# Attention and feed-forward kernel: transposes one step late, ninth blocks of two tiles together, inverse sums turned by VectorE and spread by DMA

## The reference

```python
q_pool = q.reshape(B, H, S // 2, 2, D).mean(axis=3)
scores = scale * np.matmul(q_pool, k.transpose(0, 1, 3, 2))
attn = np.exp(scores - np.max(scores, axis=-1, keepdims=True))
attn = attn / (np.sum(attn, axis=-1, keepdims=True) + 1e-09)
x = np.matmul(attn, v)                      # then (B*S/2, H*D)
h = x @ w_in
out = (np.maximum(h, 0.0) + alpha * np.minimum(h, 0.0)) @ w_out
```

## Time and profile before

| | us |
|---|---|
| median of 3 runs | 931.72 |
| the profiled execution | 932.26 |
| its span, first to last instruction | 929.7 |
| TensorE busy | 887.3 |
| VectorE busy | 516.9 |
| ScalarE busy | 423.4 |
| GpSimd busy | 213.3 |

### The profile page before, as it was taken

One profiled execution on the slowest core, in us unless ns is written; L12 is line 12 of the kernel. 1 busy time (PEld: TensorE's weight loads), 2 busy tenths in 40 slices (PEclk: granted clock), 3 DMA queues, 4 the chain that ended last, 5 costly groups with the idle time before them and its releaser, 6 DMA issues. The chain is left out here.

```text
span 929.7 us, 20770 instructions
## 1 busy us (share of the span) xinstructions
PE 887.3 (95%) x6896; PEld 623.2 (67%) x6896; DVE 516.9 (56%) x836; ACT 423.4 (46%) x963; POOL 213.3 (23%) x182
## 2 busy tenths in 40 slices
PE   3799999999999999999999999999999999999997
PEld 1455555555555555555545799989999999989995
DVE  2676767677767776767676344344444444343442
ACT  2566666666666666666666222222322222322222
POOL 2112111211121112111200323323232323323230
PEclk9999999999999999999999999999999999999999
DMA  7435423542354235523520122212422222322211
GB/s 186 106 83 135 119 65 82 133 121 63 82 133 123 60 82 133 127 57 82 133 71 1 59 68 58 67 62 63 136 57 68 57 68 61 132 59 66 65 36 68
DMA packets 36366, 79.57 MB, mean 86 GB/s; under 512 B 5360, under 2 KB 9456, under 8 KB 36336
## 3 DMA queue, kind: packets, MB, share of 16 engines
q1 hardware_dynamic: 33936, 74.48, 31.0%
q10 hardware_dynamic: 2400, 4.72, 1.5%
HBM read 74.46 MB, written 4.72 MB: 85 GB/s over the span
## 5 line engine op out<-in xcount | busy, mean ns | idle before, releaser
L432 DVE TENSOR_REDUCE neg_max<-s_ps 128x1 f32<-128x1152 f32 x144 | 194.1, 1348 | 16.6 <-DVEq L431 16.6
L573 PE MATMUL pv_ps<-pt,v_f 128*64 128x256 f32 (+1 forms) x1152 | 169.0, 414 | 0.0
L532 PE MATMUL s_ps<-k_f,q_f 64*128 64x512 f32 (+1 forms) x640 | 160.2, 626 | 5.2 <-PEq L543 5.2
L348 ACT ACTIVATE e_sb<-s_ps,neg_max 128x1024 f32<-128x1024 f32 x144 | 160.1, 1112 | 0.0
L587 PEld LDWEIGHTS slot_ps<-ident,e_sb 64*128 64x128 f32 x2304 | 86.0, 139 | 82.4 <-issue 82.4
L465 DVE COPY pt<-slot_ps 128x512 f32<-128x512 f32 x144 | 99.6, 692 | 61.3 <-DVEq L464 59.4
L341 ACT ACTIVATE e_sb<-s_ps,neg_max 128x128 f32<-128x128 f32 x144 | 52.9, 367 | 171.5 <-ACTq L340 171.5
L617 PE MATMUL slot_ps<-x_hi,wi_hi 128*128 128x384 f32 x384 | 129.5, 337 | 1.1 <-PEq L613 1.1
L617 PE MATMUL slot_ps<-x_lo,wi_hi 128*128 128x384 f32 x384 | 129.5, 337 | 0.0
L617 PE MATMUL slot_ps<-x_hi,wi_lo 128*128 128x384 f32 x384 | 129.0, 336 | 0.0
L479 DVE TENSOR_SCALAR e_sb<-slot_ps,alpha_sb 128x384 f32<-128x384 f32 x96 | 59.3, 618 | 123.2 <-DVEq L477 123.2
(11 more groups left out here) (46 smaller groups left out, 1098.8 us busy)
## 6 DMA issues: line engine op xcount, KB each, us to landing
q_raw<-in_q SPq DMA_DIRECT2D x64, 288.0 KB, 4.5
k_f<-in_k SPq DMA_DIRECT2D x64, 288.0 KB, 4.2
wi_raw<-in_w_in SPq DMA_DIRECT2D x48, 256.0 KB, 2.6
wo_raw<-in_w_out SPq DMA_DIRECT2D x48, 256.0 KB, 2.6
v_f<-in_v SPq DMA_DIRECT2D x32, 288.0 KB, 3.0
out<-pt ACTq DMA_DIRECT2D x6, 768.0 KB, 4.4
k_end<-in_k SPq DMA_DIRECT2D x64, 32.0 KB, 4.0
alpha_sb<-in_alpha SPq DMA_DIRECT2D x1, 8.0 KB, 4.7
```

The costliest lines, as they stand in the source:

```text
L348: nc.scalar.activation(e_sb[:, b * NKEY + at:b * NKEY + at + n], s_ps[:, S_AT[b] + at:S_AT[b] + at + n], ACT.Exp, bias=neg_max[:, b:b + 1] ...
L432: nc.vector.tensor_reduce(out=neg_max[:, b:b + 1], in_=s_ps[:, S_AT[b]:S_AT[b] + NKEY], op=ALU.max, axis=AX_X, negate=True).then_inc(max_r ...
L532: ins = nc.tensor.matmul(s_ps[to:to + m, S_AT[b] + at:S_AT[b] + at + BANK], q_f[2 * g + h][rows, first:first + m], k_f[2 * g + h][rows, at ...
L573: ins = nc.tensor.matmul(pv_ps[h * D:(h + 1) * D, 0:n], v_f[2 * g + h][:, a, :], pt[:, a, at:at + n], start=(a == 0), stop=(a == KT - 1))
```

## The change

Each point is a part of the diff.

- TensorE transposes tile s-1 in step s, before it waits for the exponentials of tile s, so only the big scores stand behind that wait. `e_sb` holds three tiles. One more step (s = 144) transposes the last tile.
- The ninth blocks of tiles s-1 and s, and the small scores of tiles s+2 and s+3, are made in even steps, one after the other, and copied by one VectorE copy of 256 columns. In odd steps the product follows the big scores. The maximum of an odd step also waits for the first exponential of the tile before (`even_cut_done`). Block 8 has its own place (`pt_last`) and comes first in each product; the products begin a step later.
- `spread_inverse` and ScalarE's copy of its result are gone. VectorE turns the inverse sums in blocks of 32; SyncE stores them to a DRAM tensor `sums` in four pieces, waits for these, and loads them back to 64 partitions for each head, in two transfers per group. `scale` stands at t = 1 and 6.
- `scale` writes unsplit `x_f`. `x_hi` and `x_lo` hold the 768 tokens of a pass: made by GpSimd for pass 0 after 14 pairs, and by ScalarE (`x_high`) and VectorE (`x_low`) in the last block f of a pass for the next one. The first weights are rounded one step earlier.

The core of the diff; where old lines only go, or stand in the listing above, there is a line of dots.

```diff
-    SOURCE = [[(0, 0, P, 0)], [(1, 0, P, 0)], [(0, P, P, 0)], [(1, P, P, 0)],
-              [(0, 2 * P, HALF, 0), (1, 2 * P, HALF, HALF)],
+    SOURCE = [[(0, 0, P, 0)], [(1, HALF, P, 0)], [(0, P, P, 0)], [(1, HALF + P, P, 0)],
+              [(0, 2 * P, HALF, 0), (1, 0, HALF, HALF)],
...
-    PT_AT = [0, 320, 128, 448, 256, 640, 896, 768, 1024]
-    PT_MIX = 576
+    PT_AT = [0, 384, 128, 512, 256, 640, 896, 768, 1024]
+    SUM_AT = [0, 3, 1, 4, 2, 5, 7, 6, 8]
     GROUPS = [(0, 320, 320, 0), (640, 896, 256, 320)]
     GROUP_TILES = [(0, 5), (5, 9)]
-    PRODUCT = {5: (0, (0, 1)), 6: (0, (2, 3)), 7: (0, (4, 5)), 8: (0, (6, 7, 8)),
-               0: (1, (0, 1)), 1: (1, (2, 3)), 2: (1, (4, 5)), 3: (1, (6, 7)), 4: (1, (8,))}
-    SPREAD = {6: 0, 1: 1}
-    INVERT = {4: 0, 8: 1}
-    FIRST = 6
+    PRODUCT = {6: (0, (8, 0)), 7: (0, (1, 2)), 8: (0, (3, 4)), 0: (0, (5, 6, 7)),
+               1: (1, (8, 0)), 2: (1, (1, 2)), 3: (1, (3, 4)), 4: (1, (5, 6)), 5: (1, (7,))}
+    INVERT = {5: 0, 0: 1}
+    SCALE = {1: 0, 6: 1}
+    FIRST = 7
...
-        e_sb = sb("e_sb", [P, 2 * NKEY])
+        e_sb = sb("e_sb", [P, 3 * NKEY])
         pt_flat = sb("pt", [P, KT * 2 * NQ])
...
+        pt_last = pt_flat[:, 0:2 * NQ]
+        pt = pt_flat[:, 2 * NQ:].rearrange("p (a c) -> p a c", a=KT - 1)
         neg_max = sb("neg_max", [P, 2])
         row_sum = sb("row_sum", [P, 2, TILES])
         sum_eps = sb("sum_eps", [P, TILES])
...
+        inv_sum = sb("inv_sum", [P, 32])
+        inv_t = [sb(f"inv_t{i}", [P, 32]) for i in range(2)]
+        inv_bc = sb("inv_bc", [P, NQ])
...
+        x_f = sb("x_f", [P, DT * NTOK])
+        ff = sb("ff", [P, 11776], F32R)
...
+            for s in range(FIRST, REST + 1):
...
+            def store_sums(group):
+                a, b = GROUP_TILES[group]
+                sp.wait_ge(inv_turned, 1).then_inc(inv_turned, -1)
+                for i in range(0, P, 32):
+                    sp.dma_start(sums[a * P:b * P].rearrange("(t p) -> t p", p=P)[:, i:i + 32],
+                                 inv_t[group][i + a:i + b, :]).then_inc(inv_stored, 16)
+            def spread_sums(group):
+                _, _, n, first = GROUPS[group]
+                sp.wait_ge(inv_stored, 64).then_inc(inv_stored, -64)
+                for h in range(2):
+                    row = sums[GROUPS[group][h]:GROUPS[group][h] + n]
+                    sp.dma_start(inv_bc[h * D:(h + 1) * D, first:first + n],
+                                 row.rearrange("(o n) -> o n", o=1).to_broadcast([D, n])).then_inc(inv_bc_in[group], 16)
+            def sums_and_qk(pair, g):
+                store_sums(0)
                 load_q(pair * 2)
+                spread_sums(0)
                 sp.wait_ge(k_free[g], 1).then_inc(k_free[g], -1)
                 load_k(pair * 2, 2 * g), load_k(pair * 2 + 1, 2 * g + 1)
+                store_sums(1)
                 load_q(pair * 2 + 1)
...
+                spread_sums(1)
...
+            sums_and_qk(2, 0)
+            with sp.Fori(0, NPAIR // 2 - 2) as two:
                 for g in range(2):
...
+                    sums_and_qk(two * 2 + 3 + g, 1 - g)
+                    load_v_pair(two * 2 + 2 + g, g)
...
+            def x_split(h):
+                nc.gpsimd.tensor_copy(x_part(x_hi, h), x_chunk(0, h)).then_inc(pool_self, 1)
+                pool.wait_ge(pool_self, 1).then_inc(pool_self, -1)
...
+            pool.wait_ge(x_done, NPAIR - 2)
+            x_split(0), x_split(1)
...
+                    exponential_cut(s + 1, exp_cut_done if s % 2 == 0 else even_cut_done)
+                if s > 0:
+                    act.wait_ge(tr_ready[0], 1).then_inc(tr_ready[0], -1)
+                    nc.scalar.activation(pt_half((s - 1) % TILES, 0), half_columns(slot_ps[0][:, :]),
+                                         ACT.Copy).then_inc(slot_free[0], 1)
                 if left > 0:
                     exponential(s + 1)
...
+                elif left == 0:
+                    wi_high(0)
...
+            def x_high(n, h):
+                nc.scalar.activation(x_part(x_hi, h), x_chunk(n, h), ACT.Copy).then_inc(x_hi_done, 1)
...
+            def scale(group, pair):
                 _, _, n, first = GROUPS[group]
...
+                dve.wait_ge(inv_bc_in[group], 32).then_inc(inv_bc_in[group], -32)
                 dve.wait_ge(pv_done, 2).then_inc(pv_done, -2)
...
+                nc.vector.tensor_tensor(x_f[:, bass.ds(pair * NQ + first, n)], pv_ps[:, 0:n], inv_bc[:, first:first + n],
                                         ALU.mult).then_inc(x_self, 1)
                 dve.wait_ge(x_self, 1).then_inc(x_self, -1)
                 dve.sem_inc(pv_free, 1)
...
+                if group == 1:
+                    dve.sem_inc(x_done, 1)
...
+                nc.vector.reciprocal(inv_sum[:, a:b], sum_eps[:, a:b]).then_inc(inv_self, 1)
+                dve.wait_ge(inv_self, 1).then_inc(inv_self, -1)
+                nc.vector.transpose(inv_t[group][:, :], inv_sum[:, :]).then_inc(inv_turned, 1)
             def step(s, pair, left=2):
                 t, g = s % TILES, s // TILES % 2
...
+                if t in SCALE and pair is not None:
+                    scale(SCALE[t], pair + (0 if s < 2 * TILES else 1))
+                    if SCALE[t] == 1:
+                        dve.sem_inc(v_free[1 - g], 1)
+                if s > 0:
+                    dve.wait_ge(tr_ready[1], 1).then_inc(tr_ready[1], -1)
+                    nc.vector.tensor_copy(pt_half((s - 1) % TILES, 1),
+                                          half_columns(slot_ps[1][:, :])).then_inc(slot_free[1], 1)
+                if t in INVERT and (INVERT[t] == 0 or pair is not None):
                     invert(INVERT[t])
...
+                if s % 2 == 0:
+                    dve.wait_ge(bank2_ready, 1).then_inc(bank2_ready, -1)
+                    nc.vector.tensor_copy(ninth_columns(ninth_tiles(s)),
+                                          ninth_blocks(ninth_tiles(s))).then_inc(ninth_free, 1)
                 if left > 1:
+                    if s % 2 == 1:
+                        dve.wait_ge(even_cut_done, 1).then_inc(even_cut_done, -1)
                     row_max(s + 2)
...
+                def x_low(h):
+                    dve.wait_ge(x_hi_done, 1).then_inc(x_hi_done, -1)
+                    nc.vector.tensor_tensor(x_part(x_lo, h), x_chunk(n + 1, h), x_part(x_hi, h).bitcast(F32),
+                                            ALU.subtract).then_inc(x_ready, 1)
                 def hidden(f, i, first, last):
                     unit(f, 0)
                     if n == 0 and not first:
...
+                        scale(1, NPAIR - 1)
+                    if last and not last_pass:
+                        x_low(0)
                     unit(f, 1)
+                    if last and not last_pass:
+                        x_low(1)
...
             def step(s, pair, left=2):
                 t, g = s % TILES, s // TILES % 2
...
+                if s > 0:
                     for i in range(2):
...
+                        pe.wait_ge(slot_free[i], 1).then_inc(slot_free[i], -1)
+                    for a in range(2 * CH):
+                        at = (s - 1) % 3 * NKEY + a * P
+                        for i in range(2):
+                            rows = slice(i * HALF, (i + 1) * HALF)
+                            ins = nc.tensor.transpose(slot_ps[i][:, a * HALF:(a + 1) * HALF], e_sb[rows, at:at + P],
+                                                      ident[rows, rows])
+                            if a == 2 * CH - 1:
+                                ins.then_inc(tr_ready[i], 1)
+                if left >= 0:
+                    pe.wait_ge(exp_done, 1).then_inc(exp_done, -1)
                 if left > 1:
...
+                    if s % 2 == 0:
+                        begin_scores(s + 2)
                     for ins in big_scores(s + 2):
                         ins.then_inc(s_ready, 1)
...
+                if s % 2 == 0:
+                    if left > 0:
+                        pe.wait_ge(exp_cut_done, 1).then_inc(exp_cut_done, -1)
+                    pe.wait_ge(ninth_free, 1).then_inc(ninth_free, -1)
+                    for i, tile in enumerate(ninth_tiles(s)):
+                        ins = transposed(tile, 2 * CH, s_ps[:, NINTH_AT + i * P:NINTH_AT + (i + 1) * P])
+                    if left > 1:
+                        small_scores(s + 2)
+                        begin_scores(s + 3)
+                        ins = small_scores(s + 3)
+                    ins.then_inc(bank2_ready, 1)
                 group, tiles = PRODUCT[t]
...
+                if t > 5:
+                    product(group, g, tiles)
+                elif pair is not None:
+                    product(group, 1 - g, tiles)
...
+            def hidden_unit(n, f, i, h, first):
+                if not first:
+                    pe.wait_ge(x_ready, 1).then_inc(x_ready, -1)
...
+            product(1, 1, (KT - 1,) + tuple(range(KT - 1)))
```

(41 more changed lines are left out.)

208 lines of the change are left out of this document (75 added, 133 removed).

## The result

The changed kernel takes 907.12 us (median of 4 runs, 906.08 to 909.01), beside 931.69 for the kernel before on the same chip: ratio 0.9739, 95% interval 0.9722 to 0.9756. The forecast was 918, range 907 to 931.

The account below looks back on a forecast made before the run. Attention bound by the longer of TensorE's work and a two-step loop through the engines. From 932.26: less 17.9 (pairs), 0.5 (first pair), 0.7 (end), plus 5.4 (feed-forward) gives 918.6; 918 as median, range 907 to 931.

Parts of the forecast that it names:

- The pairs: Attention's head pairs: 29.69 us each against 30.88, a gain of 1.19 a pair, 17.9 us over 15 pairs.
- I take 0 for it, and bound it at 0.1 us: TensorE's ninth blocks and small scores in rows: saving on their 0.48 us taken as 0, at most 0.1 each odd step.
- The late wait: TensorE's wait after the readout, last in the even tile's loop: 0.18 us taken, 0.44 as the upper end.
- The first pair: First pair of heads: bound by its loop before and after the change, 0.5 us gained.
- The sums' way: Inverse sums stored and loaded back by DMA: 10.0 to 13.8 us for group 0, 13.9 to spare, taken as hidden.
- Rival 4: Sums land late and scale(0) holds VectorE: 1 to 2 us a pair, 934 to 949 us; chance 0.08.
- far end for group 1: Group 1's sums by DMA, stores queued behind the k loads: at most 18.3 us, with 17 us to spare.
- The end: End of attention: wait for the first weights' split and part of the last spread go, extra steps cost; 0.7 us gained.
- The feed-forward part: x_high and x_low at pass ends delay TensorE 2.7 us a boundary, two boundaries: +5.4 us (3.9 to 7.3).
- The first gap: First of three TensorE gaps at a pass boundary: unit (15,1)'s result at 655.4, wanted at 654.59, called 0.9 us late.
- Rival 1: TensorE alone decides, the even loop being under 6.1 us: 28.9 us a pair, 906 us; chance 0.14.
- Rivals 2 and 3: 2: even loop 6.48 us, late wait 0.44, 924 us, chance 0.17; 3: loop 6.77, copy dear as 512 columns, 936, 0.11.

Follow-up runs that it names:

- no_next_x: The changed kernel without x_high and x_low for passes 1 and 2, which then read the first pass's tokens: 904.65 us, ratio 0.9719.
- copy_twice: The changed kernel with VectorE's copy of the ninth blocks made twice, first into an unused tile: 922.19 us, ratio 0.9902.
- unpaired: The changed kernel with one ninth block and one small score in every step, lag and DMA kept: 910.5 us, ratio 0.9779.
- invert_late: The changed kernel with the inversion of the sums behind the row maximum, in the same step: 916.77 us, ratio 0.984.
- the spread's slot: The changed kernel with inverse sums again spread by TensorE, which needs slot 0 that the lagging transposes have just filled: 930.83 us, ratio 0.9992.
- invert_next: The changed kernel with the inversion of the sums behind the row maximum and one step later: 910.0 us, ratio 0.9772.
- best: The changed kernel with one product block shifted, token splitting shared with GpSimd, and inversion one step later behind the maximum: 903.93 us, ratio 0.971.

## Why the forecast was right, and where it was too small

The direction and the mechanism held, the size did not. The time lies inside the range by 0.12 us, less than its own executions differ, so that it fell inside is luck; the narrower forecast, 912 to 922, missed, and the gain is nearly twice the forecast one. In the profiled executions 26.2 us went, 13.7 had been forecast. By its steps:

- **The pairs**: 17.9 forecast, 26.2 measured (1.74 for each of 15, taken from the 14 pairs between the big scores of steps 9 and 135). This is two thirds of the miss. The stretches of two steps, forecast and measured: (0,1) 6.90, 6.80; (2,3) 6.40, 6.40; (4,5) 6.24, 6.09; (6,7) 6.93, 6.91; (8,0) 7.16, 6.94; (1,2) 6.40, 6.20; (3,4) 6.24, 6.09; (5,6) 6.47, 6.40; (7,8) 6.64, 6.44. The pattern is right throughout. The mis-sized term is "I take 0 for it, and bound it at 0.1 us": four small operations in a row cost 0.79 to 0.81, not 0.96, outside that bound. This shortens TensorE's work and the loop alike by 0.15 or more in eight of nine stretches; in all the 18 steps are 1.1 us shorter than the 59.4 forecast, 8.3 us over 15 pairs. The Trainium skill ("TensorEngine Tiling (Array Packing)", Key Properties) says that changing the tiling mode drains TensorE. The trace agrees in sign: one change of mode less in two steps, 0.15 us. No run separates such a drain from the operations' own overlap.
- **The late wait**: 0.18 taken, 0.14 measured. Choosing the nearest row, not the 0.44 behind three waits, was right.
- **The first pair**: "bound by its loop in both, 0.5 gained" is not what the two traces show. Big scores of steps 0 and 9 are at 20.50 and 53.12 before, at 19.30 and 49.66 after: 3.5 gained, 1.2 of it before step 0. Part is the clock. Before, it was granted at 0.57 from 24 to 28 us, at the lower level for most of that time, which the page's slices of 23 us do not show (the prediction read the upper level in every slice from them); after, it was 1.00 there. changed_again, the same kernel as after, had it at 0.83 from 35 to 45 us, and its step 9 stands at 51.26, 1.6 later. So as an estimate up to 1.6 of the 3.5 belongs to that one execution of the kernel before. What made the rest stays open.
- **The sums' way**: hidden, as forecast. Four stores are issued in 1.3 us, not 2.4; SyncE issues the loads 2.7 to 3.0 us after the first store, and each lands in 3.6 us. Rows of one group:

```profile
300.39 1.29 SPq L251 DMA_DIRECT2D sums<-inv_t  x4
...
303.36 1.16 SPq L260 DMA_DIRECT2D inv_bc<-sums  x2
...
315.36 0.49 DVE L493 TENSOR_TENSOR x_f<-pv_ps,inv_bc 128x320 f32 x1 [0.22 <-DVEq L492]
```

From the first store to the landing of the second load it is about 7.2 us, and scale(0) comes 15 us after the first store. Rival 4 did not occur. The prediction's far end for group 1, 18.3 us, was above the 17 it had to spare, so by its own numbers "hidden" was likely and not certain. The Trainium skill ("DMA: Bandwidth & Descriptors", Anatomy of one DMA) gives its 2 us of fixed cost for DMAs that GpSimd issues, and here SyncE issues them: the estimate of 8.8 us from it is nearer to the 7.2 than my 10.0 to 13.8, but a single load took 3.6.
- **The end**: 0.7 gained was forecast, about 1.0 lost. From step 135 to the first feed-forward matmul it is 30.14 us before and 29.33 after, 0.8 gained where a pair in the middle gains 1.74. The wait of 1.05 for the first weights is gone as forecast, but TensorE waits 0.98 us at 480.94, before the ninth blocks of step 142, for an exponential; the prediction had no such term.
- **The feed-forward part**: 5.4 lost forecast, 3.3 measured, of which the boundaries are 3.4 by the traces and 2.5 to 2.8 by no_next_x's median. Its two operations were taken too long by a tenth. The first gap was also rounded up: by the prediction's own times (655.4 against 654.59) it is 0.8, and with the measured 1.47 and 1.76 it comes to 0.3, beside the measured 0.20.
- Outside the span 1.8 us lie after and 2.6 before.

Rival 1 (TensorE alone, 906) is near in time and wrong as mechanism: copy_twice adds 15 us with TensorE's work unchanged. Rivals 2 and 3 fell with 0.14 and 0.42. Rival 2's own sum was low: with a loop of 6.48 its 18 steps come to 60.35 and not 60.1, which makes 925 of its 924.

## What to carry to other kernels

Where a loop through several engines and one engine's own work are close, write down both for each stretch and take the longer; here that gave every stretch within 0.22 us. Small errors of one sign still add up: they were 8.3 us. List the one-step loops too, and what stands at the head of the next step on the engine where something is moved: three of my misses (unpaired, invert_late, the spread's slot) were by their traces a buffer or a queue place one step away. Two parts of a change may be worth more together (24.5 us) than the sum of each alone (15.3). When two traces differ in a stretch that repeats nowhere, look at the granted clock of that stretch first.

## What the runs showed of the hardware

A VectorE transposition of 128x32 in blocks of 32 takes 0.21 us. Storing the sums (0.5 KB a transfer) from SBUF to DRAM and waiting for four of them took under 3.0 us, and a broadcast load of 64 to 80 KB landed in 3.6. GpSimd subtracts 1536 columns in 3.44 us, where VectorE takes 1.76. A small VectorE operation with two inputs in SBUF took 2.02 us instead of 0.15 when it began during such a subtraction, and ended within 0.02 us of it (invert_next and best); beside one, VectorE's maximum over 1152 columns of PSUM kept its 1.35. In some traces the granted clock falls to the lower level for a short stretch between 24 and 45 us (0.57 from 24 to 28 us before, 0.83 from 35 to 45 in changed_again), in others of the same kernel not (1.00 after).
